# Column 128 of the transform for odd k carried in column 0 of the sine products, and the closing sums of the first half ordered by sign

## The reference

```python
X = np.fft.fft(X, axis=1); X = np.fft.fft(X, axis=2)
x = X.real.reshape(B * S, D)           # 12032 x 256
h = x @ moe_w_in; r = np.maximum(h, 0.0); x = (r * r) @ moe_w_out
h = x @ moe2_w_in; out = (h * np.cos(h)) @ moe2_w_out
```

## Time and profile before

| | us |
|---|---|
| median of 3 runs | 1892.62 |
| lowest and highest | 1892.49, 1892.69 |
| the profiled execution | 1893.0 |
| its span | 1891.0 |
| PE busy in the span | 1878.6 |
| PEld busy | 1580.4 |
| DVE busy | 1431.6 |
| ACT busy | 1260.5 |

### The profile page before, as it was taken

The page is one execution under the profiler, slowest core; times in us unless marked ns, Lnnn a source line. Parts: engine busy times, 40 slices in busy tenths (PEclk is TensorE's granted clock), DMA queues, the critical chain, the costliest instruction groups (busy, mean ns, idle before and its releaser), DMA issues.

```text
span 1891.0 us, 21340 instructions
## 1 busy us (share of the span) xinstructions
PE 1878.6 (99%) x8450; PEld 1580.4 (84%) x8450; DVE 1431.6 (76%) x1669; ACT 1260.5 (67%) x1324; POOL 0.2 (0%) x4
## 2 busy tenths in 40 slices
PE   8999999999999999999999999999999999999999
PEld 6888888888888888888888888888888888888887
DVE  8978877876876877777787687677677777777666
ACT  7867756765765765676676576576667667567655
POOL 0000000000000000000000000000000000000000
PEclk9999999999999999999999999999999999999999
DMA  7642112113112211100111311210000000000000
GB/s 278 252 136 85 43 64 92 40 37 123 56 53 93 64 64 68 56 6 13 44 40 36 113 56 53 86 38 6 11 23 6 12 23 6 1 22 1 1 12 22
DMA packets 37811, 105.55 MB, mean 56 GB/s; under 512 B 4296, under 2 KB 14664, under 8 KB 37456
## 3 DMA queue, kind: packets, MB, share of 16 engines
q1 hardware_dynamic: 35696, 90.27, 14.1%
q10 hardware_dynamic: 2016, 13.94, 2.1%
HBM read 85.65 MB, written 27.82 MB: 60 GB/s over the span
## 4 chain that ended last, share of the span: by engine, by line
PE 96%; DMA 1%; DVE 1%; ACT 1%; SPq 0%; issue 0%; DVEq 0%; ACTq 0%
PE ps L1010 96%; DMA stage_t<-tables 1%; DMA stage_a<-w2i 1%; DVE gh L925 0%; DVE kbuf L962 0%; ACT tab_even L566 0%; DVE u L967 0%; DVE weo L760 0%; DVE u L968 0%; PE ps L1156 0%; SPq L382 0%; SPq L379 0%; DVE gh L922 0%; DVE wo L833 0%; DVE wsp_last L754 0%
## 5 line engine op out<-in xcount | busy, mean ns | idle before, releaser
L1010 PE MATMUL ps<-gh,wo 128*128 128x502 f32 x4596 | 1089.3, 386 | 1.2 <-DVE gh L922 0.6
L1010 PEld LDWEIGHTS ps<-gh,wo 128*128 128x128 f32 x4596 | 861.7, 188 | 167.8 <-DVE gh L925 2.2
L1010 PE MATMUL ps<-y,wi 128*128 128x502 f32 x2304 | 545.4, 385 | 0.0
L1010 PEld LDWEIGHTS ps<-y,wi 128*128 128x128 f32 x2304 | 431.9, 188 | 80.5
L975 DVE TENSOR_TENSOR u<-kbuf,ps 128x1004 f32<-128x1004 int32 x192 | 230.4, 1200 | 323.7 <-ACT kbuf L735 323.6
L925 DVE TENSOR_TENSOR gh<-u,gh 128x1004 fp32r<-128x1004 f32 x383 | 458.9, 1198 | 3.5 <-ACT gh L645 1.9
L735 ACT ACTIVATE kbuf<-ps 128x1004 int32<-128x1004 f32 x192 | 193.7, 1009 | 327.2 <-PE ps L1010 327.2
L720 ACT ACTIVATE u<-u 128x1004 f32<-128x1004 f32 x192 | 200.6, 1045 | 143.4 <-DVE u L968 142.4
L1010 PE MATMUL ps<-eo,weo 128*128 128x502 f32 x1146 | 287.1, 386 | 0.0
L1010 PEld LDWEIGHTS ps<-eo,weo 128*128 128x128 f32 x1146 | 214.9, 188 | 41.0
L747 ACT ACTIVATE u<-u 128x1004 f32<-128x1004 f32 x192 | 200.4, 1044 | 65.2 <-DVE u L975 65.2
(11 more groups left out here) (103 smaller groups left out, 335.1 us busy)
## 6 DMA issues: line engine op xcount, KB each, us to landing
ring<-scratch_t SPq DMA_DIRECT2D x72, 378.0 KB, 4.0
xin<-x SPq DMA_DIRECT2D x36, 512.0 KB, 3.3
out<-io SPq DMA_DIRECT2D x23, 502.0 KB, 3.4
scratch_t<-tables ACTq DMA_DIRECT2D x12, 756.0 KB, 4.7
io<-scratch_eo SPq DMA_DIRECT2D x11, 502.0 KB, 4.6
scratch_eo<-est SPq DMA_DIRECT2D x14, 376.5 KB
stage_t<-tables SPq DMA_DIRECT2D x6, 756.0 KB, 15.8
tab_odd<-scratch_t ACTq DMA_DIRECT2D x2, 2268.0 KB, 11.6
```

The source lines that it names most:

```text
L1010: op = pe.matmul(out_, a, b, start=start and i == 0, stop=stop and i == len(todo) - 1)
```

## The change

- The column 128 for odd k goes into the sine products. The sum for it needs a cosine sum over s; in the sine product it is done on values taken at Q - s (`x128` and `lx` get a second half for them; `mirror128` holds the result), and the signs of every second k are turned afterwards. Before, column 0 of the sine rows was unused.
- Product (None, 0, 1) is gone, and with it its 18 matmuls, its `take_rows`, its ScalarE copy and its store. `lastc` and `lfold` are half as large.
- `sum_odd(1)` and step 2 of `rows_fold` for sine write column 0 from `mirror128` first, and the other 127 columns as before.
- `take_rows` of a product (b, 1, 1) ends with two multiplications by -1 on one partition, with a wait between them.
- `store_rows` of (b, 1, 1) also stores row 0 to `scratch_a`; `load_a` waits for that.
- `load_raw` is two transfers, the cosine part with 128 rows and the sine part with rows 1 to 127. Row 0 of the sine part in `raw` is set to zero once, in tile 0.
- At the first flush the sums of sign 0 of both waiting chunks come first, then those of sign 1.
- Steps from tile 0's mix chunks on have a number c smaller by one, so the two buffers of `hb` change places.

```diff
-PRODUCTS = [(None, 0, 0), (0, 0, 0), (0, 1, 0), (0, 1, 1), (None, 0, 1), (0, 0, 1)]
+PRODUCTS = [(None, 0, 0), (0, 0, 0), (0, 1, 0), (0, 1, 1), (0, 0, 1)]
-EARLY, BESIDE, INSIDE = 3, 5, 6
+EARLY, BESIDE, INSIDE = 3, 4, 5
...
-    items += [Item("row", r=3), "flush", Item("row", r=4)]
+    items += [Item("row", r=3), "flush"]
...
         def load_a(t):
+            b, j = divmod(t, TB)
+            if j:
+                sp.wait_ge(est_st, 16 * stores_until(number[b, 1, 1]))
...
-            sp.dma_start(raw[:, :, :], scratch_eo[b, :, :, j * T:(j + 1) * T].rearrange("e p k -> p e k")).then_inc(
-                raw_in, 16)
+            at_ = slice(j * T, (j + 1) * T)
+            sp.dma_start(raw[:, 0, :], scratch_eo[b, 0, :, at_]).then_inc(raw_in, 16)
+
+            sp.dma_start(raw[1:P, 1, :], scratch_eo[b, 1, 1:P, at_]).then_inc(raw_in, 16)
...
+                if phase and odd:
+                    sp.dma_start(scratch_a[b:b + 1, at_], est[0:1, 0:KP]).then_inc(est_st, 16)
...
-            act.wait_ge(raw_in, 16 * t)
+            act.wait_ge(raw_in, 32 * t)
+            act.wait_ge(raw_zeroed, 1)
...
-            dve.tensor_tensor(odd_rows[phase], odd_terms[0], odd_terms[1],
+            if phase:
+                dve.wait_ge(mirrored128, 1)
+                dve.tensor_copy(odd_rows[phase][:, :, 0:1], mirror128[:, :, 0:1])
+            dve.tensor_tensor(odd_rows[phase][:, :, phase:], odd_terms[0][:, :, phase:], odd_terms[1][:, :, phase:],
                               ALU.subtract if phase else ALU.add).then_inc(odd_sum, 1)
...
+            elif phase and odd:
+
+                subtract_rows(r, 0, mirrored).then_inc(mirrors_done, 1)
+                dve.tensor_scalar(to[0:1, 1:n:2], to[0:1, 1:n:2], -1.0, None, ALU.mult)
+                dve.wait_ge(mirrors_done, b + 1)
+                dve.tensor_scalar(to[0:1, n:n + mirrored:2], to[0:1, n:n + mirrored:2], -1.0, None,
+                                  ALU.mult).then_inc(rows_out, 1)
...
-                dve.tensor_tensor(fold[:, 1, :], xin[:, 0, 0, :], xin[:, 1, 0, :], ALU.subtract).then_inc(folded, 1)
+                if phase:
+                    dve.wait_ge(mirrored128, 1)
+                    dve.tensor_copy(fold[:, 1, 0:1], mirror128[:, 2 * kt + parity, b:b + 1])
+                dve.tensor_tensor(fold[:, 1, phase:], xin[:, 0, 0, phase:], xin[:, 1, 0, phase:],
+                                  ALU.subtract).then_inc(folded, 1)
...
+                if it.t == 0 and it.index == 8:
+                    dve.wait_ge(est0_st, 16)
+                    dve.memset(raw[0:1, 1, :], 0.0).then_inc(raw_zeroed, 1)
...
-                for old in waiting:
-                    if old is steps[-1]:
-                        last_down()
-                    else:
+                if steps[-1] in waiting:
+                    for old in waiting[:-1]:
                         down(old)
+                    last_down()
+                else:
+
+                    for sign in range(2):
+                        for old in waiting:
+                            down(old, [sign])
```

More of the change, by code:

```diff
@@ L180, in program @@
     ab, *w128 = area(A_AB, A_F, ("ab", [P, T], F32), ("w128_0", [P, NF // 2], F32))
-    est, *w128_1 = area(A_F + 26496, end, ("est", [P, EW], F32), ("w128_1", [P, NF // 2], F32))
+    est, *w128_1 = area(A_F + 26496, end, ("est", [P, EW], F32), ("w128_1", [P, NF // 2], F32),
+                         ("mirror128", [P, 2 * KT, B], F32))
+    mirror128 = w128_1.pop()
     w128 += w128_1
@@ L220, in program @@
         for name, first in (("odd_rows", A_F), ("odd_terms", A_F + 6144))]
[L222 to L223 removed]
+    wrow0, lsum, lfold = area(A_GH + 37888, A_OSB, ("wrow0", [P, WP], F32), ("lsum", [P, 2, 2 * KT, 2, B], F32),
+                              ("lfold", [P, 2 * KT, B], F32))
+    wrow = [wrow0] + area(A_WO1 + 28672, A_WI2, ("wrow1", [P, WP], F32), ("wrow2", [P, WP], F32))
     wrow.append(wrow[1])
@@ L290, in stores_until @@
     def stores_until(r):
-        return r - 1 if r >= EARLY else 1
+        return 1 + sum(1 + (PRODUCTS[i][1:] == (1, 1)) for i in range(EARLY, r + 1))
     def fold_step(it):
@@ L838, in _ @@
         for i in range(2):
-            dve.memset(lastc[i][:, 4 * KT * B:].bitcast(F32), 0.0).then_inc(zeroed, 1)
+            dve.memset(lastc[i][:, 2 * KT * B:].bitcast(F32), 0.0).then_inc(zeroed, 1)
         dve.wait_ge(lx_in, 16)
-        dve.tensor_tensor(lsum[:, :, :, :], lx[:, :, 0:2, :], lx[:, :, 2:4, :], ALU.add).then_inc(lsummed, 1)
+        dve.tensor_tensor(lsum[:, :, :, :, :].rearrange("p m t j b -> p (m t) j b"),
+                          lx[:, :, :, 0:2, :].rearrange("p m t j b -> p (m t) j b"),
+                          lx[:, :, :, 2:4, :].rearrange("p m t j b -> p (m t) j b"), ALU.add).then_inc(lsummed, 1)
         dve.wait_ge(lsummed, 1)
-        for odd in range(2):
-            dve.tensor_tensor(lfold[:, odd, :, :], lsum[:, :, 0, :], lsum[:, :, 1, :],
-                              ALU.subtract if odd else ALU.add).then_inc(lfolded, 1)
+        dve.tensor_tensor(lfold[:, :, :], lsum[:, 0, :, 0, :], lsum[:, 0, :, 1, :], ALU.add).then_inc(lfolded, 1)
+        dve.tensor_tensor(mirror128[:, :, :], lsum[:, 1, :, 0, :], lsum[:, 1, :, 1, :],
+                          ALU.subtract).then_inc(mirrored128, 1)
         dve.wait_ge(last_hi, 1)
-        dve.tensor_tensor(lastc[1][:, 0:4 * KT * B], lfold[:, :, :, :].rearrange("p e t b -> p (e t b)"),
-                          lastc[0][:, 0:4 * KT * B].bitcast(F32), ALU.subtract).then_inc(last_lo, 1)
+        dve.tensor_tensor(lastc[1][:, 0:2 * KT * B], lfold[:, :, :].rearrange("p t b -> p (t b)"),
+                          lastc[0][:, 0:2 * KT * B].bitcast(F32), ALU.subtract).then_inc(last_lo, 1)
         dve.wait_ge(c_hi, 1)
@@ L1162, in last_down, with down @@
             op.then_inc(g_used, 1)
-        def down(it):
+        def down(it, signs=range(2)):
             place = it.n % 2
@@ L1172, in down @@
                     pe.wait_ge(split_lo, order.index(("o1", it.index // 2)) + 1)
-                for sign in range(2):
+                for sign in signs:
                     if it.n == 0 and sign == 1:
@@ L1188, in down @@
                         op.then_inc(y1_sum, 1)
+                if 1 not in signs:
+                    return
             else:
@@ L1249, with with_folded @@
     s = np.minimum(2 * np.arange(KT * P).reshape(KT, 1, P) + np.arange(2).reshape(1, 2, 1), Q)
-    x = np.stack([x[:, s], x[:, H - s], x[:, (S - s) % S], x[:, H + s]], axis=4)
-    x128 = np.ascontiguousarray(x[..., P].transpose(3, 1, 2, 4, 0).reshape(P, 2 * KT, 4, B))
+    def with_folded(a, s):
+        return np.stack([a[:, s], a[:, H - s], a[:, (S - s) % S], a[:, H + s]], axis=4)
+    x128 = with_folded(x[..., P], np.stack([s, Q - s]))
+    x128 = np.ascontiguousarray(x128.transpose(5, 1, 2, 3, 4, 0).reshape(P, 2, 2 * KT, 4, B))
+    x = with_folded(x, s)
     mirrored = np.concatenate([x[..., 0:1], x[..., D - 1:P:-1]], axis=-1)
```

33 lines of the change are left out of this document (15 added, 18 removed).

## The result

The changed kernel takes 1926.2 us (median of 4 runs, 1925.2 to 1927.8), the kernel before beside it 1892.6 us: a ratio of 1.0179, 95% interval 1.0162 to 1.0197. It is slower by 33.7 us. The forecast was 1913.7 us with a range of 1904 to 1938, and one of its rivals, a clock that falls after each stall, gave 1926. The profiled execution took 1927.8 us, with a span of 1925.8.

What follows compares the result with a forecast made beforehand. TensorE was taken as the bound, busy 1794.00 of 1794.00 us from 92 to 1886 us. Terms 20.0 + 3.5 + 0.5 - 2.9 = +21.1 us; 1893.0 + 21.1 - 0.4 = 1913.7 us, range 1904 to 1938.

Steps and rivals of the forecast that it cites:

- One engine carries the 127 rows: Sine-part loads: 127 rows have no equal shares, so one DMA engine carries all of them, 10.2 us a load.
- Rival A: Sine loads: rows dealt unequally over 16 engines, nothing late, only -2.9 us stays, 1889.7 us; chance 0.10.
- 80 ns a row: Sine loads: one engine at 25 GB/s takes 80 ns for each row; 73 and 95 ns as the other values.
- The x load late, and what TensorE loses: Tiles 1, 3, 4, 6 and 7: x load 4.7 us late, TensorE loses 4.0 us each, 20.0 us in all.
- Rival B: Sine loads: one engine carries the rows but later transfers don't wait for them, about 1891 us; chance 0.04.
- The threshold, 69 rows: Sine loads: with up to 69 rows on the busiest engine, nothing is late.
- Tile 2: Last three ring loads of tables go behind the sine rows, the last landing about 461 us: +3.5 us.
- Tile 1's own load: Tile 1's row load shares its engine with copies of tables: +0.5 us, 0 to 2.
- The 18 products: Half of tile 0: 18 matmuls less on TensorE, -3.1 us, with nothing taken as lost behind them.
- The cover at the half: Half of tile 0: split first sums ready at 106.42, closing sums end at 106.64, 0.2 us of cover.
- VectorE in tile 0 and the first load: First half of tile 0: VectorE's added copy and memset +0.2 us; the doubled first load +0.05 us.
- rival C: As forecast, but TensorE's clock falls after each of six stalls, 2 us each, +12 us: 1926 us; chance 0.14.

Runs made afterwards that it cites:

- 97: The changed kernel with the sine part's 127 rows loaded as 97 and 30 rows: 1901.9 us.
- 83 rows: The changed kernel with the sine part's 127 rows loaded as 83 and 44: 1895.4 us in ten second-time runs; first time, two of four lay at 1895, two at 1911.
- kernel with 112 and 15 rows: The changed kernel with the sine part's 127 rows loaded as 112 and 15 rows: 1889.8 us, ratio 0.9985 to the kernel before.
- the old order: The changed kernel with sine rows loaded as 112 and 15, and the first half's closing sums ordered chunk by chunk as before: 1890.9 us.
- the kernel before with a load of 127 rows: The kernel before with only its row load split: 128 cosine rows, sine rows 1 to 127, and sine row 0 alone: 1928.8 us, ratio 1.0193.
- 106 + 21: The changed kernel with the sine part's 127 rows loaded as 106 and 21 rows: 1889.6 us, ratio 0.9984 to the kernel before.

## Why the prediction was right, and where it was off

- **One engine carries the 127 rows.** Right: one completion, 25 GB/s, and the same for 97 and 83 rows (in 157 to 176 us 64 small packets = 48 + 1 + 15, and 60 = 48 + 1 + 11); two engines for 106. Of the rule cited from the Trainium skill ("DMA: Bandwidth & Descriptors", section "Why a DMA increments its semaphore by 16 and not by 1"), all counts of this case agree: 1, 2, 7, 15 and 16 completions for 127, 106, 21, 15 and 112 rows. Rival A is out.
- **80 ns a row.** Right: 81 ns by the three row counts. The 95 ns taken from the earlier trace rows as the upper end was a mean over mixed transfers.
- **The x load late, and what TensorE loses.** 4.7 us late and 4.0 us lost in each of five tiles were forecast; 5.1 and 20.4 / 5 = 4.1 us came, the latter being 4.10, 4.39, 3.95, 4.10 and 3.85 us. That the loss came out so close is in part luck. The x load landed 12.7 us after its issue, where the forecast had 175.8 - 163.61 = 12.2. And the slack was 1.0 us (5.14 - 4.10), not 0.7: the forecast had TensorE's next product of `eo` and `weo` wait for u, but that product ran at 171.53 as if nothing were late, and the one that stood was of `gh` and `wo`, for `gh`. The two misses cancel. Rival B is out by the waits for x, five times 5.1 us. The threshold, 69 rows, is 64 by the runs.
- **Tile 2.** This term was mis-sized: TensorE stood for 1.78 + 0.15 = 1.9 us before the ring products, in place of 3.5. But the forecast counted the end of the nine products, and by that measure it was nearly right for a reason that it did not have. From 460.6, where they were due, to 465.37, where the next ones start, are 4.8 us in place of 1.6, so 3.2 us were lost; the clock fell at 463.06, and half speed for the last six products took about 1.0 of them. The three ring loads, issued from 454.20 on, landed after 8.1, 8.5 and 9.0 us, the last at about 464.2 us, 15.7 us after the load of rows was issued at 448.50. The forecast had 16.4. TensorE had no wait for the last one, since at half clock it was still busy with the second. At the full clock the last three products would have ended at about 464.8 in place of 462.2: an estimate of 2.6 us for the term. That it landed 0.7 us early goes back to the start of the sine rows, taken as 3.1 us after the issue (3.7 from tile 1, where an output store runs ahead, less 0.6). The DMA view from 441.5 to 466 us, in slices of 0.61 us, has the steady 25 GB/s from 450.7 on, 2.2 us after.

```profile
GB/s 0 0 123 331 365 390 227 324 409 290 79 0 7 164 249 23 26 26 26 23 26 26 125 334 399 313 225 354 191 51 33 30 25 25 25 30 5 0 0 0
```

- **Tile 1's own load.** Forecast 0.5 us; no stall is there. (With 127 rows in the cosine part too it was 10.25 us.)
- **The 18 products.** -3.1 us were forecast with nothing lost behind them; the trace gives 106.52 against 109.77, of which 0.12 us came earlier, so -3.1. In this trace 0.2 us of it is lost again at once: the 24 matmuls behind take 5.60 us, where before they took 5.36. The kernel with 112 and 15 rows shows no such loss (106.55 to 111.93), so it does not belong to the change. The cover at the half was 0.2 us as worked out: 105.05 + 1.26 = 106.3 against 106.5, and the old order, without cover, cost 1.1 us.
- **VectorE in tile 0 and the first load.** Forecast +0.25; TensorE reaches the closing sums at 100.92 where it was 101.04 before. The copy and the memset took 0.17 and 0.48 us, as priced, and they were felt: behind the memset TensorE waits 0.16 us for `gh` at 74.30, and a lead of 0.48 us over the kernel before shrinks to 0.14. The lead is none of the change's doing as far as can be seen; the kernel before with a load of 127 rows, the same up to here, has 0.4 us of it. At 91 us both kernels wait, 0.39 us before and 0.23 now, and start 0.11 us apart, so the wait took up the rest, as the forecast said. What the doubled first load costs is too small to be seen beside such differences.
- **The change without its load.** The trace of the kernel with 112 and 15 rows has 106.55 against 109.77, -3.2 us, and the medians say -2.5. The interval of that ratio, 0.9976 to 0.9994, is -4.5 to -1.1 us and holds both. The traced run of the kernel before, 1893.0, lay 0.7 us above its median of 1892.3, which is the size of the difference.
- **The clock.** Here the forecast itself failed. Its sum has no term for the clock, because no stall was in the trace before; I gave that case 0.14 as rival C. With the terms as measured, the forecast's sum is 20.4 + 1.9 - 2.5 = +19.8 us, 1912 us; the 14 us from there to 1926.2 are the stretches at half clock, 14.7 us by the table above. Rival C said 2 us for each of six stalls, 12 us; it was 1.5 to 1.7 (tiles 4 and 2) to 3.1 us. That its 1926 is the measured time is luck in part: its terms for stalls were some 1.3 us too high together, and its clock was 2.7 us too low. Its reason, as long as the stall, is not the law: 1.5 to 3.1 us came after stalls of 1.8 to 4.4 us, 2.7 us after one of 13.1, nothing after the five stalls up to 1.0 us with 83 rows nor after 1.5 to 1.95 us with 97. The arithmetic for such a stretch is that of the Trainium skill ("TensorE: Matmul & The Clock Gate", section "HAM oscillation — how this bites in real kernels"): half of the time spent at 1.2 GHz is lost. The trace agrees: 15 matmuls in 6.05 us at 0.50, 29 in the next 6.05 at 1.00.

```profile
177.13:183.18 6.05, 6.05 (x15) 4.84 (x16) 3.71 (x7) 3.64 (x4) 0.00 (x0) 0.50 0.20 64
183.18:189.23 6.05, 6.05 (x29) 5.08 (x28) 4.35 (x7) 4.45 (x6) 0.00 (x0) 1.00 0.06 22
```

The mechanism was right and the measured time lay in the range; the point value was low since a known rival was treated as an alternative to the forecast where it is a surcharge on it: if TensorE stands for 4 us, the question is only what the clock does next, and 0.14 was too little for that.

## What to carry to other kernels

Before a transfer loses a row, count how its rows divide: 127 of 128 put ten microseconds of work on one DMA engine, and everything behind it in the queue waits; 112 + 15 or 106 + 21 cost nothing here, and a queue of its own took away the stalls behind the x loads. Price a stall of TensorE of about 2 us or more at its length plus what the half clock behind it may cost, 1.5 to 3 us each where the clock fell here. A removal of work that pays 2.5 us is worth having, but only once every transfer that was reshaped for it has been looked at in the DMA view.

## What the runs showed of the hardware

- The clock fell after stalls of 1.78 us (tile 2 of the changed kernel), of 2.41 us and of every longer one, and not after 1.95 or 1.50 us, so the length of the stall alone does not decide. In the changed kernel's stalls of about 4 us it fell 2.1 to 3.7 us after TensorE stopped, in the 13 us stall of tile 1 4.9 us after; in two stalls of 4.2 us of the kernel before with 127 rows it fell only when TensorE ran again. In the changed kernel it stayed at half for 3.4 us (tiles 2 and 4) or 6.8 us (tiles 1, 3, 6 and 7), and for 13.6 us in and behind the 13 us stall.
- An engine with two queues serves them in turn: 127 rows in one, on it until 171.4 us, did not keep eight rows of the other from landing by 168.1 us. They landed 2.8 us later than with the rows spread, though.
- Rows on one engine can hold up the issuing too. Behind two loads of 127 rows SyncE was busy for 9.9 us with issuing the x load, which takes it 0.34 us behind one.
- TensorE was once 4% slower for hundreds of microseconds at a granted clock of 1.00. In the first run of the 83 rows, from 1560 to 1890 us with no stall near it, it did 1416 matmuls where the second run did 1479, with the same DMA load; at the same work that is 15 us, and the spans of the two, 1908.7 and 1893.6 us, differ by as much. The kernel before had such runs beside it too, 1919.3 us for one, so it is not the kernel's. Its start was at no event that the trace shows, and its cause is open. The pace itself, 233 ns from one matmul to the next in place of 223, is seen elsewhere too: the 24 closing sums at the half of tile 0 take 5.60 us, 233 ns each, in the traces of both kernels. The rows, first and second run:

```profile
1560.00:1890.00 330.00, 330.00 (x1416) 271.56 (x1415) 225.29 (x231) 205.50 (x207) 0.00 (x0) 1.00 0.02 8
```

```profile
1560.00:1890.00 330.00, 330.00 (x1479) 276.99 (x1477) 233.62 (x238) 212.87 (x215) 0.00 (x0) 1.00 0.02 8
```
